# Q, K and V laid out before the launch, and the first products of the next stage interleaved with attention

## The reference

```python
# attention, for each batch and head
k_sum = k.reshape(B, H, 24, 32, 64).max(axis=3)
v_sum = v.reshape(B, H, 24, 32, 64).mean(axis=3)
local = scale * q @ k.T          # masked to |i - j| < 16
block = scale * q @ k_sum.T + log(32)
a = softmax(concat([local, block]))
x = a @ concat([v, v_sum])       # then (2, 768, 512)
# MoE
h = relu(x @ w_in)                               # 512 -> 1024
conv = sum(conv_w[k] * shift(h, k - 1) for k in range(3))   # along the sequence
x = (h * sigmoid(conv)) @ w_out                  # 1024 -> 512
# second block
xn = (x - mean) / sqrt(var + 1e-6) * g_ln
out = x + relu(xn @ w_ch1) @ w_ch2               # 512 -> 2048 -> 512
```

## Time and profile before

| | us |
|---|---|
| median of three runs | 462.5 |
| profiled execution, first to last instruction (span) | 460.9 |
| PE busy | 452.0 (98%) |
| PE weight loads busy | 400.5 (87%) |
| DVE, ACT, POOL busy | 275.0, 200.1, 268.3 |

### The profile page before, as it was taken

The page is one execution under the profiler, slowest core; times in us unless marked ns, Lnnn a source line. Parts: engine busy times, 40 slices in busy tenths (PEclk is TensorE's granted clock), DMA queues, the critical chain, the costliest instruction groups (busy, mean ns, idle before and its releaser), DMA issues.

```text
span 460.9 us, 8619 instructions
## 1 busy us (share of the span) xinstructions
PE 452.0 (98%) x3114; PEld 400.5 (87%) x3114; DVE 275.0 (60%) x630; ACT 200.1 (43%) x503; POOL 268.3 (58%) x405
## 2 busy tenths in 40 slices
PE   7899999999999999999999999999999999999997
PEld 6687888989989889989889988998998899889885
DVE  4999976876666967974674254546762244124333
ACT  3898997433335746436243143422421233123210
POOL 2559689999945000097898889750042687878000
PEclk9999999999999999999999999999999999999999
DMA  9998951212102000002115324120020211220003
GB/s 229 213 232 197 195 140 53 92 47 91 47 0 93 0 1 0 1 0 91 54 41 143 109 93 93 67 91 1 26 89 23 93 46 47 91 93 0 1 0 137
DMA packets 74725, 35.28 MB, mean 77 GB/s; under 512 B 57632, under 2 KB 68924, under 8 KB 74684
## 3 DMA queue, kind: packets, MB, share of 16 engines
q1 hardware_dynamic: 71164, 33.85, 27.1%
q10 hardware_dynamic: 3520, 0.88, 0.9%
HBM read 28.83 MB, written 3.15 MB: 69 GB/s over the span
## 4 chain that ended last, share of the span: by engine, by line
PE 96%; DMA 1%; DVE 1%; issue 1%; ACT 1%; ACTq 0%; DVEq 0%
PE two L1689 10%; PE two L1687 10%; PE two L1688 10%; PE two L1664 9%; PE two L1667 8%; PE two L1666 8%; PE two L1460 5%; PE two L1462 5%; PE two L1461 5%; PE two L1595 5%; PE two L1596 5%; PE two L1594 5%; PE two L1413 3%; PE two L1445 3%; PE two L1424 3%; PE two L1342 3%
## 5 line engine op out<-in xcount | busy, mean ns | idle before, releaser
L640 POOL TENSOR_TENSOR asum<-wst 128x256 f32<-128x256 f32 x26 | 21.8, 838 | 93.4 <-PE two L1462 50.2
L1664 PE MATMUL two<-combo,wa 128*128 128x384 f32 x224 | 75.8, 338 | 0.0
L1667 PE MATMUL two<-combo,wa 128*128 128x384 f32 x224 | 75.6, 337 | 0.0
L1666 PE MATMUL two<-combo,wa 128*128 128x384 f32 x224 | 75.2, 336 | 0.0
L1689 PE MATMUL two<-wv,h 128*128 128x512 f32 x192 | 75.0, 391 | 0.0
L1687 PE MATMUL two<-wv,h 128*128 128x512 f32 x192 | 74.8, 390 | 0.2 <-DVE h L946 0.2
L1688 PE MATMUL two<-wv,h 128*128 128x512 f32 x192 | 75.0, 390 | 0.0
L1023 DVE TENSOR_TENSOR u<-two,u 128x384 f32<-128x384 f32 x16 | 8.9, 558 | 90.2 <-PE two L1667 90.2
L1267 ACT ACTIVATE h<-u 128x384 fp32r<-128x384 f32 x16 | 8.4, 525 | 122.4 <-DVE u L1023 122.4
L574 POOL TENSOR_SCALAR pn<-ex,rinv 128x120 f32<-128x120 f32 x96 | 34.8, 383 | 19.1 <-DVE rinv L736 18.4
L634 POOL TENSOR_TENSOR wa<-asum,wa 128x256 fp32r<-128x256 f32 x52 | 43.2, 831 | 4.3
(11 more groups left out here) (119 smaller groups left out, 981.0 us busy)
## 6 DMA issues: line engine op xcount, KB each, us to landing
wst<-in_moe_w_ch SPq DMA_DIRECT2D x26, 512.0 KB, 3.2
vW<-in_v SPq DMA_DIRECT2D x13, 288.0 KB
kn<-in_k SPq DMA_DIRECT2D x15, 192.0 KB, 3.8
qn<-in_q SPq DMA_DIRECT2D x15, 192.0 KB, 3.7
out<-y SPq DMA_DIRECT2D x11, 256.0 KB, 2.0
wst<-in_moe_w_in SPq DMA_DIRECT2D x8, 256.0 KB, 3.1
wst<-in_moe_w_out SPq DMA_DIRECT2D x8, 256.0 KB, 2.8
tok<-xq SPq DMA_DIRECT2D x32, 48.0 KB, 2.0
```

The costliest lines, as they stand in the source:

```text
L1664: nc.tensor.matmul(o, wk[:, 0, kk], ck[:, 0, kk], start=(first and kk == 0), stop=False, skip_group_check=True)
L1666: nc.tensor.matmul(o, wk[:, 0, kk], ck[:, 1, kk], start=False, stop=False, skip_group_check=True)
L1667: ins = nc.tensor.matmul(o, wk[:, 1, kk], ck[:, 0, kk], start=False, stop=(kk == 1), skip_group_check=True)
```

## The change

`kernel()` now lays out the inputs on the host side of the call: q and k as (pair, 128, seq) with the head dimension first, k with 16 zero columns on both sides; v as (pair, seq, 128) with 16 zero rows on both sides; `g_ln` and `conv_w` as the columns that the kernel wants. No instruction turns K, Q or the vectors any more:

- K of the pairs 1 to 7 is loaded by one DMA each straight into the windows (`kW`, 384 B pieces, overlaps included); Q is one DMA (3072 B per partition); V is one DMA of 512 B pieces. K and Q have three buffers each instead of two.
- K of pair 0 comes in three plain pieces into `kT0`; ACT copies them into windows (`first_window_keys`), DVE takes the maxima of each piece. `key_max` of the other pairs reads the windows in SBUF.
- `keys_t`, `queries_t`, `window_keys`, `queries`, the transpose of `rows` and four warm-up transposes are gone. `block_keys`, `block_means`, `load_vsum` stay.
- The turned probabilities have two banks in turn up to group 11 (`probs_at`).
- Each `exps` waits for its own `score_max` and not for all four.
- All lists are new. Chunks 0 to 5 of `hidden` and chunks 0 to 3 of `project` stand in them (`LISTED = 6`), from behind `scores(15)` on; `sigmoid(0)` stands before `exps(19)`. 14 splits of weights stand ahead of the last `normalise` instead of 8. The loops begin at s = 6.

PE at the start of the program, before. Names are those of the tiles: `kn` and `qn` are K and Q as loaded, `kW` and `qT` the operands of the scores, `vW,means` is `block_means`, `ident,pn` is `probs_t`.

The core of the diff, without the lists:

```diff
@@ names and sizes
+    SP = S + 2 * WIN
+    LATE = GPP * PPB
+    FIRST = GT + 2 * WIN
+    LISTED = 6
...
+        def k_windows(p, b0, nb):
+            a = k[p, :, 0:1]
+            return bass.AP(a.tensor, a.offset + QB * b0, [[SP, P], [QB, nb], [1, KEYS]])
+        def v_windows(p):
+            a = v[p, 0:1]
+            return bass.AP(a.tensor, a.offset, [[P, KEYS], [QB * P, NQ], [1, P]])
+        def probs_at(n):
+            return bank[6] if n < LATE and n % 2 else bank[2]
@@ SP
             def load_k(p):
-                if p >= 2:
-                    sp.wait_ge(ktr_ready, p - 1)
-                b, hp = p // PPB, p % PPB
-                for h in range(2):
-                    sp.dma_start(kn[:, p % 2, :, h],
-                                 k[b, 2 * hp + h].rearrange("(t p) d -> p t d", p=P)).then_inc(kn_in[p % 2], 16)
+                if p >= 3:
+                    sp.wait_ge(s_ready, GPP * (p - 2))
+                sp.dma_start(kW[p % 3][:, :, 0:KEYS], k_windows(p, 0, NQ)).then_inc(k_in[p % 3], 16)
+            def first_k():
+                for g in range(GPP):
+                    c = slice(GT * g + (FIRST - GT if g else 0), GT * g + FIRST)
+                    sp.dma_start(kT0[:, c], k[0, :, c]).then_inc(k_first_part(g), 16)
             def load_q(p):
...
+                sp.dma_start(qT[p % 3][:], q[p]).then_inc(q_in[p % 3], 16)
             def load_v(p):
...
-                for dst, src in v_parts(p):
-                    sp.dma_start(dst, src).then_inc(v_in[p % 3], 16)
+                sp.dma_start(vW[p % 3][0:KEYS], v_windows(p)).then_inc(v_in[p % 3], 16)
+            first_k()
+            sp.dma_start(qT[0][:, GT:S], q[0, :, GT:S]).then_inc(q_in[0], 16)
             load_k(1)
             load_q(1)
+            load_v(0)
+            load_v(1)
             load_k(2)
+            load_vsum(0)
             load_q(2)
...
@@ DVE
+            def first_key_max():
+                for g in range(GPP):
+                    dve.wait_ge(k_first_part(g), 16)
+                    nc.vector.tensor_reduce(out=ks[:, 2 * GB * g:2 * GB * (g + 1)],
+                                            in_=kT0[:, WIN + GT * g:WIN + GT * (g + 1)].rearrange("p (n i) -> p n i", i=BLK),
+                                            op=ALU.max, axis=AX.X).then_inc(ks_done, 1)
...
             def key_max(p):
-                dve.wait_ge(ktr_ready, p + 1)
...
+                dve.wait_ge(k_in[p % 3], chunk_in(p))
+                dve.wait_ge(ksb_done, p)
...
@@ ACT
             def exps(n):
-                act.wait_ge(mx_done, GB * (n + 1))
...
                 for j in range(GB):
+                    act.wait_ge(mx_done, GB * n + j + 1)
@@ PE
             def hidden(s, parts=range(8)):
                 b, c = s // KF, s % KF
+                if parts[0] == 0:
+                    pe.wait_ge(w_done, w_ready("in", c))
+                if s == 0 and parts[0] == 0:
+                    pe.wait_ge(pts_done, LATE)
+                    pe.wait_ge(x_done, GPP * PPB)
...
-            for s in range(2, 2 * KF):
+            for s in range(LISTED, 2 * KF):
```

More of the change, by code:

```diff
@@ L890, in _ @@
             x_low(23)
+            taps(2)
+            gate(2)
+            taps(3)
+            gate(3)
+            taps(4)
+            taps(5)
+            gate(4)
+            gate(5)
             def stats(i):
@@ L1561, in _ @@
-            probs_t(18)
-            scores(22)
-            outputs(17)
-            block_means(7)
-            probs_t(19)
-            scores(23)
-            outputs(18)
-            hidden(0, [4, 5])
-            probs_t(20)
-            hidden(0, [6, 7])
-            outputs(19)
-            probs_t(21)
-            hidden(1, range(KD))
-            outputs(20)
-            hidden(1, range(KD, 2 * KD))
-            probs_t(22)
-            outputs(21)
-            probs_t(23)
-            outputs(22)
@@ L1598, in project @@
                     ins.then_inc(tile_proj, 1)
+            pe.wait_ge(pool_link, IDENT_LINKS)
+            warm(13)
+            scores(0)
+            scores(1)
+            scores(2)
+            block_means(0)
+            scores(3)
+            probs_t(0)
+            probs_t(1)
+            scores(4)
+            block_means(1)
+            probs_t(2)
+            scores(5)
+            outputs(0)
+            outputs(1)
+            scores(6)
+            probs_t(3)
+            outputs(2)
@@ new lines, in _ @@
+            scores(7)
+            block_means(2)
+            probs_t(4)
+            scores(8)
+            probs_t(5)
+            outputs(3)
+            scores(9)
+            outputs(4)
+            outputs(5)
+            scores(10)
+            probs_t(6)
+            block_means(3)
+            probs_t(7)
+            scores(11)
+            outputs(6)
+            outputs(7)
+            probs_t(8)
+            probs_t(9)
+            scores(12)
+            outputs(8)
+            block_means(4)
@@ new lines, in _ @@
+            scores(13)
+            probs_t(10)
+            outputs(9)
+            probs_t(11)
+            scores(14)
+            outputs(10)
+            outputs(11)
+            block_means(5)
+            scores(15)
+            hidden(0, [0, 1, 2, 3])
+            scores(16)
+            probs_t(12)
+            hidden(0, [4, 5, 6])
+            probs_t(13)
+            hidden(0, [7])
+            outputs(12)
+            outputs(13)
+            scores(17)
+            probs_t(14)
+            hidden(1, [0, 1])
@@ new lines, in _ @@
+            probs_t(15)
+            hidden(1, [2])
+            scores(18)
+            block_means(6)
+            hidden(1, [3])
+            outputs(14)
+            outputs(15)
+            scores(19)
+            probs_t(16)
+            hidden(1, [4, 5, 6])
+            probs_t(17)
+            hidden(1, [7])
+            hidden(2, [0, 1])
+            scores(20)
+            outputs(16)
+            outputs(17)
+            hidden(2, [2])
+            scores(21)
+            probs_t(18)
@@ new lines, in _ @@
+            hidden(2, [3, 4])
+            block_means(7)
+            probs_t(19)
+            hidden(2, [5])
+            scores(22)
+            hidden(2, [6, 7])
+            outputs(18)
+            outputs(19)
+            scores(23)
+            probs_t(20)
+            hidden(3, [0, 1, 2, 3, 4])
+            probs_t(21)
+            hidden(3, [5])
+            project(0, [0])
+            outputs(20)
+            outputs(21)
+            probs_t(22)
+            project(0, [1])
+            hidden(3, [6])
@@ new lines, in _ @@
+            probs_t(23)
+            hidden(3, [7])
+            outputs(22)
+            outputs(23)
+            hidden(4, [0])
+            project(0, [2])
+            project(0, [3])
+            project(0, [4])
+            hidden(4, [1, 2, 3])
+            project(0, [5])
+            project(1, [0])
+            project(1, [1])
+            project(1, [2])
+            project(1, [3])
+            project(1, [4])
+            project(1, [5])
+            hidden(4, [4, 5])
+            project(2, [0])
@@ L1600, in tokens_t @@
+            project(2, [1])
+            hidden(4, [6, 7])
+            hidden(5, [0, 1])
+            project(2, [2])
+            project(2, [3])
+            project(2, [4])
+            project(2, [5])
+            project(3, [0])
+            hidden(5, [2, 3, 4])
+            project(3, [1])
+            project(3, [2])
+            hidden(5, [5, 6, 7])
+            project(3, [3])
+            project(3, [4])
+            project(3, [5])
             def tokens_t(slot, dst):
```

652 lines of the change are left out of this document (270 added, 382 removed).

## The result

The changed kernel took 471.31 us (median of four runs, 470.65 to 472.42) where the one before took 462.93 in runs on the same chip: a ratio of 1.0182, with a 95% interval of 1.0160 to 1.0204. It is 8.4 us slower, not 7.8 us faster, and outside the range. The 96 turns of K and Q are gone and yet the first product of MoE stands at 47.39 us, 7.1 us later than forecast.

What follows compares the result with a forecast made beforehand. Transfers through K5 were to set hidden(0)'s start, PE's work the rest: 40.3 + 400.05 + 10.0 moved work + 0.8 changes + 2.0 waits = 453.15 us span, 454.7 with 1.6 around it, 7.8 us less; range 448.5 to 460.5.

Steps and rivals of the forecast that it cites:

- The end of the lists: After attention's last group: long products and moved weight splits, 11 us ahead of the old list, costed at nothing.
- the gate of chunk 4: Suspected, with the weights, if the first product comes by 41 us yet the gain is under 3 us; nothing allowed.
- The price of the transfers: Loads up to K5: 9.78 MB, K and V at 279 GB/s, 288 overall, putting K5 at 36.6 us.
- The chain behind them: DVE after K5: its maximum, score_max(14), x_low(9) to (11) and a cast, 3.7 us; hidden(0) starts at 40.3.
- ACT's chain: From exps(3) at 13.6 us, ACT's work at 89% busy leads to x_low(11), ending at 39.4 us.
- The idle time: Start-up and waits of PE ahead of hidden(0), said to stay about the 12 us they were.
- The work moved behind the first product: Scores, means, probs_t and outputs now left for PE after hidden(0) starts: 10.0 us more there.
- the changes at 0.1 us: PE switching between fast products and scores, outputs or means: 16 such changes instead of 8, +0.8 us.
- The mixed stretch: From hidden(0) to outputs(23): PE 39.5 us, ACT 40.5 at 89%, plus 2.0 us of waits taken.
- The first: Rival: K and V pieces move at no more than 222 GB/s, hidden(0) at 50.5, kernel 464.9 us; chance 0.07.
- The second: Rival: ACT works only 75% of the mixed stretch, 8.5 us of waits, 461.2; chance 0.08 shared with transfers at 228 to 248.
- The fourth: Rival: PE's 11.4 us of turns only filled gaps DVE and ACT make, so nothing gained; no separate chance.

Runs made afterwards that it cites:

- the runs with plain K: Changed kernel, tail order mended, K loaded without overlaps, POOL copying the windows: 0.9967; with V on 128 partitions and the loads reordered too: 0.9891.
- the best version: Changed kernel with tail order mended, loads reordered, V on 128 partitions, K loaded without overlaps and POOL copying its windows: 458.32 us, ratio 0.9891.
- the run with fewer bytes: Changed kernel loading only one of twelve V windows for pairs 3 to 7, all instructions kept: 468.18 us, ratio 1.0125.
- V cured: New layout with the lists of before, less turns and copies, and V loaded onto 128 partitions instead of 96: 462.29 us, ratio 0.9977.

## Why the prediction was wrong

**The end of the lists, costed at nothing: 5.6 us of time, shown.** "I cost them at nothing; PE's slack against them is what hides them": the step failed. I had followed the order only as far as the last group of attention. One `tap0` behind a `relu` that waits for the next chunk emptied PE for 4.0 us, and the clock took 2.3 more. Taking it out gave 5.6 us of time by the ratios, and 6.5 us behind the first product between the two profiles. The prediction named the gate of chunk 4 as the place, under a condition that wasn't met.

**The price of the transfers, shown in part.** I took 279 GB/s for K and V between two rows, as if a piece's size were all, 288 with the rest. Up to 42 us the changed kernel moved 247, and K5, for which I had 36.6, was in at 42.3 by the packet records:

```profile
2.70:42.00 39.30, 30.75 (x538) 23.49 (x538) 25.62 (x158) 26.89 (x116) 20.24 (x60) 0.78 0.99 247
```

V's share of that ran at 249 for want of partitions, whatever the size of its pieces, which is below even the 282 GB/s of the 256 B pieces of before. Another part is a queue that ran short while SP waited (206 and 219 GB/s from 15 to 25 us), which the sum had not at all: SP issued K5 only at 38.26. K was not slow per byte (315 GB/s at 5 to 10 us, with Q and the first of V among it), but its overlaps are half as many bytes again, and taking them out was worth 3.3 to 4.4 us (the runs with plain K against those without). By the rule of the Trainium skill ("DMA: Bandwidth & Descriptors", § Specifications) on transfers under 512 B, K's pieces would fall short of line rate and V's reach it. In the changed kernel the rows have it the other way round, K at 315 GB/s and V at 249; with V on 128 partitions both were near 350 (340 at 5 to 10 us, 347 at 10 to 12), so the rule decided nothing here.

**The chain behind them.** By my step the transfers decide through K5. `key_max(5)` began at 43.29 with no wait for a load:

```profile
43.29 0.95 DVE L720 TENSOR_REDUCE ks<-kW 128x24 f32<-128x768 f32 x1
```

The 3.7 us from there to `x_low(11)` roughly held (it ended at 46.5), but loads struck much earlier: V0 at 11.96 (for 10.9), Q3 at 30.14. From 30.14 on PE had no gap but 0.60 us, for V5, until 47.39. The lists are in order, so what came late at 30 us was late at 47. The sum had two chains that end at K5 or on ACT, and none through PE's own list.

**The start.** First `exps` 7.05 for 6.3; fourth 16.04 for 13.6. In the best version the fourth is at 15.85, with no wait of PE for V0, so these 2.3 us are not V's doing. Its lines on ACT:

```profile
15.37 0.59 ACT L1093 COPY pts<-two 120x512 f32<-120x512 f32 x1 [1.29 <-PE two L1425]
15.85 0.40 ACT L1083 ACTIVATE ex<-sm,mx 128x120 f32<-128x120 f32 x1
```

My sum had `scores(3)` at 11.7; there it began at 13.22, because `scores(1)` and `(2)` had waited 1.22 and 1.10 us for maxima and the groups went at the lower pace (the means held PE for 1.44 us and not 0.79). From its start to `exps(3)` I had 1.87 us, and it took 2.63: `exps(3)` stands behind `probs_out(0)` in ACT's list, and that waits for `probs_t(0)`, which PE does behind `scores(3)`. With these 2.3 us ACT's chain gives 39.4 + 2.3 = 41.7, and the best version has 43.13.

**The idle time, that I had "stay about the 12 us".** PE's work ahead of the first product is 48.9 - 11.4 - 10.0 = 27.5 us. The changed kernel needed 47.4, so 19.9 are not work at full pace: 4.6 before the first wait (5.91 - 1.30), 9.1 of waits, and some 5.7 by half clock (about 13 us of PE at 1.01 for 0.57), which leaves 0.5.

**What held.** The work moved behind the first product, the changes at 0.1 us and the mixed stretch. 412.85 was forecast for what stands behind the first product; with the tail mended it was 414.95, with the loads in another order as well 413.8, and in the best version 413.3. The mixed stretch was 43.0 us for 41.5. The timeline of PE shows the price of a change, 0.26 where the next products go at 0.17, answering to the earlier trace rows:

```profile
49.41 0.34 PE L1448 MATMUL two<-xT,win 128*128 128x384 f32 x1
49.67 0.64 PE L1394 MATMUL two<-kW,qT 64*64 64x120 f32 x16
```

**The rivals.** The first (transfers no faster, 464.9) was right that the transfers would be late: 247 GB/s, just under the 248 from which it decides, and waits for V. But its path, K5 and then `key_max(5)`, was not the one that bound, as far as the run with fewer bytes shows, and PE's longest wait was for Q3. Its first product was to come at 50.5 and came at 47.39; the time is worse than it said because of the tail. Its chance of 0.07 was too low. The second, ACT at 75%, did not occur. The fourth, turns that were covered anyway, has its outcome in the layout with the old lists (1.0036, and 0.9977 with V cured) but only in part its mechanism: new waits and PE's slower pace, and not gaps that DVE and ACT had made before.

**What stays open.** Of the 16.6 us between forecast and result the best version gets back 13.0. Why V on 96 partitions slows stretches in which K and Q move is not explained, nor why the loads come later in one profile than in another of the same lists. What the slower pace of PE's first 16 us costs once the loads are mended was not tested.

## What to carry to other kernels

Price a transfer by its shape as well as its piece: count partitions, and count the bytes that overlapping windows load twice, since an idle engine may make the windows for less. When lists are written out by hand, follow each engine's to its very end, and ask of every waiting instruction what stands behind it. An issuing engine's list is such a list too: a load behind a wait comes late however fast it then moves. Work taken from an engine is time only if nothing else comes late in its place and the engine keeps its clock; judge the clock by how long a known group holds PE.

## What the runs showed of the hardware

- A load onto 96 partitions moved 249 GB/s with 512 B pieces and 255 with 6144 B; onto 128 partitions 347 and 431. With 256 B pieces it made no difference (282 and 277 in windows with K and Q among them; 18 ns a piece in both).
- The DMA share of a window goes to 1.28, so 1.00 doesn't mean that no more could be moved: 222 GB/s stood at 0.99 and 282 at 1.25, with the same pieces.
- In the changed kernel gaps of PE of 1.30 and 1.22 us close together, or one of 3.2 or 4.0, came with a granted clock of 0.50 for 7 to 10 us. With turns of the identity in the first gaps it stayed at 1.00 there.
- A granted clock given as 1.00 may only mean that there is no record: in the best version the records begin at 15.9 us, and from 6.29 on, behind a gap of 1.67, groups of scores held PE for 1.01 us where at 2.4 GHz they hold it for 0.57.
